# A fused kernel in twelve units of 256 rows in place of eight of 384

## What is computed

```python
k_n = k / (np.linalg.norm(k, axis=-1, keepdims=True) + 1e-06)
for t in range(S):                                  # 768 steps, for 4 x 8 heads
    y[:, :, t] = q[:, :, t] @ state
    v_old = state^T k_n[t]
    state = state + beta[t] * outer(k_n[t], v[t] - v_old)
x = y as rows of (4 * 768, 384)
x = (sigmoid(x @ w_gate) * (x @ w_val)) @ w_out     # 384 -> 1536 -> 384
out = x.copy()
rows with x @ w_skip > 0: e = argmax(x @ w_gate2)
    out = x + softmax(x @ w_gate2)[e] * (relu(x @ w1[e]) @ w2[e])   # 384 -> 1024 -> 384
```

## Time and profile before

| | |
|---|---|
| median of 3 runs | 981.93 us |
| profiled execution, its own time | 981.73 us |
| its span in the trace | 979.7 us |
| TensorE busy | 946.7 us (97%) |
| VectorE busy | 450.5 us (46%) |
| ScalarE busy | 165.1 us (17%) |
| GpSimd busy | 104.6 us (11%) |
| substitution on VectorE (L636, L638) | 79.2 + 79.8 us |
| dense products on TensorE (L1079, L1088, L1099) | 204.9 + 204.7 + 206.1 us |
| DMA over the span | 78.75 MB, mean 80 GB/s |

### The profile page before, as it was taken

The page is one execution under the profiler, slowest core; times in us unless marked ns, Lnnn a source line. Parts: engine busy times, 40 slices in busy tenths (PEclk is TensorE's granted clock), DMA queues, the critical chain, the costliest instruction groups (busy, mean ns, idle before and its releaser), DMA issues.

```text
span 979.7 us, 23053 instructions
## 1 busy us (share of the span) xinstructions
PE 946.7 (97%) x10087; PEld 629.2 (64%) x10087; DVE 450.5 (46%) x1100; ACT 165.1 (17%) x346; POOL 104.6 (11%) x136
## 2 busy tenths in 40 slices
PE   5999999999999999999999999999999999999995
PEld 5965655666565566566556655665555578878874
DVE  7967754766567457536753673212012211211121
ACT  2121211121121131122112111211110021111110
POOL 2010100011010010101010101001001222222221
PEclk9999999999999999999999999999999999999998
DMA  8830004003100400040031000000910115551400
GB/s 351 319 115 2 26 19 146 26 3 116 57 18 2 176 13 1 20 168 2 2 118 71 1 2 34 18 1 18 374 46 0 60 35 195 204 198 50 156 26 28
DMA packets 30299, 78.75 MB, mean 80 GB/s; under 512 B 4072, under 2 KB 20120, under 8 KB 29312
## 3 DMA queue, kind: packets, MB, share of 16 engines
q1 hardware_dynamic: 20112, 61.46, 17.2%
q10 hardware_dynamic: 6912, 9.55, 2.7%
q0 software_dynamic: 3184, 6.39, 2.2%
HBM read 65.34 MB, written 13.00 MB: 80 GB/s over the span
## 4 chain that ended last, share of the span: by engine, by line
PE 93%; DVE 2%; DMA 2%; issue 1%; POOL 1%; SPq 0%; ACT 0%; ACTq 0%; DVEq 0%; POOLq 0%
PE ps L1099 21%; PE ps L1079 19%; PE ps L1088 19%; PE ps L1152 9%; PE ps L1164 9%; PE ps L940 3%; PE ps L982 2%; PE ps L1038 2%; DMA prod<-in_turned_moe_w_out 1%; PE ps L1012 1%; PE ps L954 1%; PE ps L997 1%; PE ps L966 1%; PE ps L1027 1%; PE ps L1044 1%; PE ps L1137 1%
## 5 line engine op out<-in xcount | busy, mean ns | idle before, releaser
L1099 PE MATMUL ps<-wo,prod 128*128 128x393 f32 x576 | 206.1, 503 | 4.8 <-DVE prod L692 4.7
L1079 PE MATMUL ps<-xT,shared 128*128 128x384 f32 x576 | 204.9, 492 | 0.7 <-ACT xT L859 0.7
L1088 PE MATMUL ps<-xT,shared 128*128 128x384 f32 x576 | 204.7, 492 | 0.0
L692 DVE TENSOR_TENSOR prod<-sig,ps 128x384 f32<-128x384 f32 x96 | 52.9, 554 | 233.5 <-PE ps L1088 232.8
L1099 PEld LDWEIGHTS ps<-wo,prod 128*128 128x128 f32 x576 | 104.5, 189 | 76.5 <-DVE prod L692 8.6
L1079 PEld LDWEIGHTS ps<-xT,shared 128*128 128x128 f32 x576 | 106.7, 190 | 70.2 <-issue 0.8
L1088 PEld LDWEIGHTS ps<-xT,shared 128*128 128x128 f32 x576 | 106.9, 190 | 69.8
L1152 PEld LDWEIGHTS ps<-xgT,arena 128*128 128x128 f32 x816 | 93.7, 192 | 5.1 <-ACT xgT L887 0.8
L1152 PE MATMUL ps<-xgT,arena 128*128 128x128 f32 x816 | 94.0, 275 | 0.6 <-ACT xgT L887 0.6
L864 ACT ACTIVATE sig<-ps 128x384 f32<-128x384 f32 x96 | 47.1, 490 | 272.9 <-PE ps L1079 272.9
L1164 PE MATMUL ps<-arena,hT 128*128 128x384 f32 x272 | 90.5, 486 | 0.0
(11 more groups left out here) (171 smaller groups left out, 707.9 us busy)
## 6 DMA issues: line engine op xcount, KB each, us to landing
arena<-in_moe_w SPq DMA_DIRECT2D x16, 1536.0 KB, 10.6
arena<-in_kq SPq DMA_DIRECT2D x7, 1536.0 KB, 8.3
x_scratch<-x ACTq DMA_DIRECT2D x24, 196.5 KB, 4.1
arena<-in_kn SPq DMA_DIRECT2D x8, 576.0 KB, 4.8
shared<-in_v SPq DMA_DIRECT2D x8, 576.0 KB, 9.5
arena<-in_kr SPq DMA_DIRECT2D x8, 576.0 KB, 4.5
out<-x ACTq DMA_DIRECT2D x24, 192.0 KB, 4.2
prod<-in_turned_moe_w_out SPq DMA_DIRECT2D x1, 2304.0 KB, 12.9
```

Source lines behind the costliest of these rows:

```text
L692: nc.vector.tensor_tensor(prod[:, f, :], sig[:, f % 2, :], ps_m[3 - f % 2][:, 0:CT], ALU.mult)\
L1079: last = nc.tensor.matmul(ps_m[f % 2][:, 0:CT], wg[:, a, f * P:(f + 1) * P], xT[:, a, :], start=(a == 0), stop=(a == KT - 1))
L1088: last = nc.tensor.matmul(ps_m[3 - f % 2][:, 0:CT], wv[:, a, f * P:(f + 1) * P], xT[:, a, :], start=(a == 0), stop=(a == KT - 1))
L1099: last = nc.tensor.matmul(ps_m[t][:, 0:XW], prod[:, a, t * P:(t + 1) * P], wo[:, a, :], start=(a == 0), stop=(a == NF - 1))
```

## The change

A unit is now one chunk (JS = 1) of all four sequences (SEQ = 4), 256 rows; there are Q = 12 units, and one state runs through all of them. NS, the number of blocks in the lanes, goes from 24 to 16 of 32, and TT from 3 to 2. Each unit has one scan step with copies twice as wide. The Gram products of a unit stand in one burst (gk, then gq), x_turn is one burst. Keys for the norms have a tile of their own (`kn`) and no longer go through the lanes; the masking factors have one too (`fac`), and the diagonal blocks are copied into the lanes by four ScalarE copies in place of a ScalarE copy and a VectorE operation. The next substitution may begin right behind from_lanes, since the pieces of the order now carry costs in us, and what is left of a substitution when 18 us of dense pieces remain is given out at once. SyncE loads keys and queries on 48 partitions for each half, without padding.

The rows below are for one engine each, in its own order; "x3" is three equal instructions.

The diff, cut to its core:

```diff
-JS = 3
-SEQ = 2
+JS = 1
+SEQ = 4
-ROOT_MIN = 1e-15
+ROOT_MIN = 1e-30
+DENSITY = 0.8
+COST = {"gate": 1.29, "val": 1.29, "out": 2.03}
...
+    def follow(us):
+        owed[1] += us
+        while behind and owed[1] > 0:
+            event, w = behind.pop(0)
+            owed[1] -= w
+            order.append(event)
+        owed[1] = min(owed[1], 0.0)
+    def piece():
+        event = pieces.pop(0)
+        order.append(event)
+        us = COST.get(event[0], 0.0)
+        follow(DENSITY * us)
+        return us
+    def dense(us):
+        owed[0] += us
+        while pieces[0][0] != "x_turn" and (owed[0] > 0.5 or pieces[0][0] not in COST):
+            owed[0] -= piece()
+    def substitution(q):
+        return [(("turn_in", q, 0), 2.1)] +             [(("solve", q, u), 0.41 + 0.0021 * u * (H2 - 1 - u)) for u in range(1, H2 - 1)] + [(("from_lanes", q, 0), 5.3)]
...
+    order += [("norm", 0, 0), ("gk", 0, 0), ("lengths", 0, 0), ("mask", 0, 0), ("gq", 0, 0), ("mask", 0, 1)]
+    order += [("turn_in", 0, 0), ("router", 0, 0), ("gk", 1, 0), ("gq", 1, 0), ("warm", 0, 10)]
+    order += [event for event, _ in substitution(0)[1:]]
...
     for c in range(Q):
         q = c + 1
+        pieces += dense_pieces(c, Q, NF, TT)
         owed[0] = 0.0
         if q < Q:
+            if q + 1 < Q:
+                behind.insert(0, (("norm", q + 1, 0), 1.9))
+                dense(6.5)
+                order += [("gk", q + 1, 0), ("gq", q + 1, 0), ("pt", q + 1, 0)]
+                behind[0:0] = [(("lengths", q + 1, 0), 0.9), (("mask", q + 1, 0), 0.7), (("mask", q + 1, 1), 0.7)]
+            while ("from_lanes", q, 0) not in order:
+                if left() > 18.0:
+                    piece()
+                else:
+                    order.append(behind.pop(0)[0])
+            if q + 1 < Q:
+                behind += substitution(q + 1)
+            dense(2.2)
             order.append(("off", q, 0))
+            dense(1.9)
             order.append(("off", q, 1))
+            dense(1.9)
+            for stage in ("read", "apply", "write"):
+                order.append((stage, q, 0))
+                dense(1.6)
+        while pieces:
+            piece()
...
         load_kn(0)
-        load_first(0)
-        load_first(1)
-        load_first(2)
+        load_first(0, k_first)
         sp.dma_start(bt[:], beta_d).then_inc(beta_in, 16)
+        load_first(1, q_first)
...
         for q in range(2, Q):
             sp.wait_ge(y_done, JS * (q - 1))
+            load_kq(q)
+            load_kn(q)
             load_kr(q)
-            load_kq(q)
             load_v(q)
-            sp.wait_ge(dt_ready, q)
-            load_kn(q)
...
             elif stage == "turn_in":
+                if q:
+                    dve.wait_ge(dt_ready, q)
                 nc.vector.transpose(bl[:], bp[:])
...
+            elif stage == "gk":
+                act.wait_ge(gk_done, q + 1)
+                nc.scalar.activation(by_group(graw[:, q % 2]), grams(ps_a[:, 0:2]), ACT.Copy).then_inc(graw_copied, 1)
+                act.wait_ge(graw_copied, q + 1)
+                if q:
+                    act.wait_ge(turned_in, q)
+                for part in range(4):
+                    block = slice(H2 * part, H2 * (part + 1))
+                    last = nc.scalar.activation(dg[block, 0:NS, :], graw[block, q % 2, :, H2 * (part % 2):H2 * (part % 2 + 1)], ACT.Copy)
+                last.then_inc(dg_ready, 1)
...
+            if stage in ("gk", "gq"):
+                a = int(stage == "gq")
+                if q == 0:
+                    pe.wait_ge((k_first, q_first)[a], 32)
+                else:
+                    pe.wait_ge(kq_in[q % 2], 32 * ((q + 1) // 2))
...
             elif stage == "val":
                 if f >= 2:
                     pe.wait_ge(prod_ready, NF * q + f - 1)
-                elif f == 1 and q:
-                    pe.wait_ge(x2_copied, TT * q)
+                elif f == 0 and q >= 2:
+                    pe.wait_ge(rank_read, q - 1)
```

More of the change, by code:

```diff
@@ L50, in dense_pieces, with program_order @@
                 pieces += [(stage, q, 0) for stage in early.get((t, part), ())]
-            if t == TT - 1 and part < 3 and q + 1 < Q:
-                pieces.append(("x_turn", q + 1, part))
-    return pieces
-def program_order(Q, QS, NF, TT, KT):
-    light = ("route", "rank", "x_turn", "logits", "logit_turn")
-    order, pieces, later = [], [], []
+            if t == TT - 1 and part == 1 and q + 1 < Q:
+                pieces.append(("x_turn", q + 1, 0))
+    return pieces
+def program_order(Q, NF, TT):
+    order, pieces, behind = [], [], []
     owed = [0.0, 0.0]
[L66 to L69, removed]
+    def follow(us):
+        owed[1] += us
+        while behind and owed[1] > 0:
+            event, w = behind.pop(0)
             owed[1] -= w
@@ new lines, in program_order @@
+    order += [("turn_in", 0, 0), ("router", 0, 0), ("gk", 1, 0), ("gq", 1, 0), ("warm", 0, 10)]
+    order += [event for event, _ in substitution(0)[1:]]
+    order += [("router_copy", 0, 0), ("off", 0, 0), ("warm", 1, 1), ("pt", 0, 0), ("off", 0, 1), ("norm", 1, 0), ("warm", 1, 2)]
+    order += [("apply", 0, 0), ("warm", 1, 1), ("write", 0, 0), ("warm", 1, 1), ("x_turn", 0, 0), ("warm", 1, 2)]
+    order += [("lengths", 1, 0), ("mask", 1, 0), ("mask", 1, 1), ("pt", 1, 0)]
+    behind += substitution(1)
@@ L119, in program_order @@
             order.append(("off", q, 0))
-            dense(1.2)
+            dense(1.9)
             order.append(("off", q, 1))
[L122 to L126, removed]
-                dense(0.7)
-                later = prepare(q + 1)
-            steps = scan(q)
-            gap = max(0.7, (sum(p[0] not in light for p in pieces) - 4.0) / len(steps))
@@ L131, in program_order @@
-            for step in steps:
-                order.append(step)
-                dense(gap)
-        order += pieces
+            dense(1.9)
[4 more added lines that the diff above has]
+            piece()
     return order
@@ L309, in program @@
     kq_in = [sem(f"kq_in{i}") for i in range(2)]
-    kq_first = [sem(f"kq_first{i}") for i in range(3)]
+    k_first = sem("k_first"); q_first = sem("q_first")
     v_in = [sem(f"v_in{i}") for i in range(2)]
@@ new lines, in att @@
+                    pe.wait_ge((k_first, q_first)[a], 32)
+                else:
+                    pe.wait_ge(kq_in[q % 2], 32 * ((q + 1) // 2))
+                if q == 1:
+                    pe.wait_ge((graw_copied, raw_copied)[a], 1)
+                elif q and a == 0:
+                    pe.wait_ge(st_ready, writes(q - 2))
+                elif q:
+                    pe.wait_ge(xt_copied, q - 1)
+                for j in range(JU):
+                    for g in range(G2):
+                        for h in range(HH):
+                            n, to = ((G2 * j + g, h), (HH * j + h, g))[a]
+                            for c in range(CG):
+                                part = slice(GP * c, GP * c + D)
+                                last = nc.tensor.matmul(
+                                    ps_a[rows(to), 2 * a + c, n * C:(n + 1) * C], kq[part, q % 2, 0, j, g, h, :],
+                                    kq[part, q % 2, a, j, g, h, :], start=True, stop=True)
```

270 lines of the change are left out of this document (106 added, 164 removed).

## The result

The changed kernel takes 1000.48 us, the median of four runs from 999.11 to 1004.18, against 980.6 us for the kernel before (four runs of the same comparison, 978.76 to 982.52): a ratio of 1.021 with a 95% interval of 1.017 to 1.025. I had forecast 982.4 us, with 971 to 993 as the range: the time lies above the range, and "slower" had a chance of 0.26.

What follows compares the result with a forecast made beforehand. The order of TensorE's own work was taken to set the dense stretch. Start -15.7 and dense stretch +16.4 (work -4.9, waits and pace +21.3), end nothing, gave +0.7 on 981.73: 982.4 us, range 971 to 993.

Steps and rivals of the forecast that it cites:

- Unit 0's stop, 10.7: In unit 0, the output product waits for column block 11 behind substitution steps and leaving the lanes: 10.7 us.
- The off stops, 1.8, 1.4 and 1.9: In units 1 to 3, TensorE waits before the first off product while the lanes are left: together 5.1 us.
- Eleven seams, 11.5: Between value 11 and the first output, every seam waits for the last product: 0.74 or 1.25 each, 11.5 us.
- All waits together: In the dense stretch, unit 0, off and seam stops sum to 27.3 us against 8.0 before: +19.3.
- Slow pace after the stop, +2.0: After unit 0's stop, about 4 us of dense work run at half speed: +2.0 us (none to 4).
- Bursts, 0.4 us each, -12.4: In the dense stretch, bursts of small products fall from 106 to 75, at 0.4 us each: -12.4 us.
- small products: In the dense stretch, small-product records go from 5,978 to 6,406 at 14.5 ns each: +6.2 us.
- The start, -15.7: Before the first gate: fewer bytes, Gram and warm-up records and scan steps bring it to 52.2 us: -15.7.
- Rival 3: At the start, weights arrive as late and warm-up is all slow: -11.5 in place of -15.7, 986.6 us; chance 0.1.
- The end: nothing: From the last rank on, a list late by 1.5 us is hidden by the gather's wait for saved rows: nothing.
- Rival 1, the waits don't come: In the dense stretch, unit 0's stop, its restart and off stops are missing: 964.6 us, half 973.5; chance 0.22.
- Rival 2, VectorE bounds every unit: In mid-unit, VectorE falls behind and costs TensorE 1.3 us in each of ten units: 995.4 us; chance 0.18.

Runs made afterwards that it cites:

- experiment 2: Changed kernel with unit 0's threshold for the rest of the substitution loosened from 18.0 to 8.2 us: 1000.58 us, ratio 1.021.
- experiment 5: Changed kernel with the thresholds of both first units loosened, 8.2 us in unit 0 and 13.0 in unit 1: 994.9 us, ratio 1.013.
- experiment 6: Changed kernel with the output stage's first three quarters waiting for eleven products only, the last for the twelfth: 986.6 us, ratio 1.006.
- Experiment 4: Changed kernel with more dense work (3.9 for 2.2 us) ahead of the first off product in units 1 to 3: 995.24 us, ratio 1.016.
- experiment 7: Changed kernel with the Gram burst split in two, a dense piece between, in ten units: 1003.97 us, ratio 1.023.
- experiment 1: Changed kernel with all transposes of a turn ahead of all its products of halves, same instructions: 993.2 us, ratio 1.013.
- Experiment 3: Changed kernel with keys and queries padded to 128 partitions, one transfer in place of two on 48: 1000.29 us, ratio 1.020.
- experiment 8: Changed kernel with the edits of experiments 1, 4, 5 and 6 together: 973.11 us, ratio 0.992.
- experiment 9: Kernel of experiment 8 with the padded 128-partition loads of experiment 3 as well: 971.1 us, ratio 0.991.
- experiment 10: Kernel of experiment 9 with a dense piece ahead of each remaining wait and thresholds 9.5 and 14.5 us: 964.7 us, ratio 0.986.

## Why the prediction was wrong, point by point

- *Unit 0's stop, 10.7.* Right: 10.06 idle, at the place and put down to the operation that was named. Experiments 2, 5 and 6 show that the block of steps ahead of the last product makes it.
- *The off stops, 1.8, 1.4 and 1.9.* Right: 4.9 in three (said: 5.1). Experiment 4 takes 3.8 of it away.
- *Eleven seams, 11.5.* Too high: 8.8. The steady one waits 0.97, which is 1.14 with its loss of pace (604.58 to 607.01, less a piece of 1.295), where I had 1.25. My sum had a slip too: five at 0.74 and six at 1.25 are 11.2. The mechanism (three steps ahead of the last product) is seen in experiment 7, whose steady unit has two there and waits 0.61.
- All waits together: said +19.3 (27.3 with their pace, against 8.0), measured +18.6 of idle time. **So the waits aren't what was missed.**
- *Slow pace after the stop, +2.0.* Right for the first: 4.16 us (100.12 to 104.28) for the 2.09 behind a steady seam (607.01 to 609.10), +2.1. Not foreseen: the short stops can have it too. Behind the stop of 1.65 in unit 1 the two off bursts and the value piece between them took 1.6 us more (5.20 from 154.57 to 159.77, for 3.62 from 575.70 to 579.32).
- *Bursts, 0.4 us each, -12.4.* A little high: 0.36 by experiment 7, so -11.2 for 31: +1.2, of which 0.8 without the turn bursts.
- *The turn burst.* **This is the step that failed**, inside the terms "small products" and "bursts". I took its records at the 14.5 ns of all small products and its burst price at the 0.4 us of the others; by that, ten bursts fewer save 4.0 us and twelve records more cost 0.2, so -3.8. Measured: 21 bursts took 13.1 us before and eleven take 20.5 now, +7.4. The forecast is short by 11.2 us here. With the kinds of record sorted the eleven take 11.0 (experiment 1), so 9.5 of the 11.2 come from the alternation inside the burst, which the full diff and the kernel show and to which no row of before that I had taken gives a price. Before, the bursts held one form each, and moving them together brought the forms side by side. Why the sorted burst still takes 1.7 us more in all than my prices give isn't settled.
- *The start, -15.7.* It came out at -11.4, and "I am wrong if the first gate comes after 56" has happened, at 56.47. The router started 5.2 us later than said (20.19 for 15.0). I had counted fewer bytes at the old rate of 424 GB/s; the rate was 230 from 12 to 20 us. Experiment 3 gives back 3.7 of the 5.2 with more bytes on more partitions. The warm-up was 2.1 shorter than said (4.5 us for 6.6), and from off to the first gate it took 12.6 and not 11.5, of which 0.9 is the turn burst. Rival 3 had -11.5 as its price, with the chance 0.1. That it is so near to -11.4 is luck: it had the weights as late as before and a warm-up that is all slow, and they came 2.9 us later than before, with a warm-up at full pace from its second record on.
- *The end: nothing.* Right: 8.9 us from the last output record to the first expert product, before (776.12 to 785.03) and after (795.03 to 803.90).
- *Rival 1, the waits don't come:* refuted. *Rival 2, VectorE bounds every unit:* no value piece waited for a product; the only other waits for VectorE in the dense stretch are two before apply products, of 1.0 us together. Its 995.4 lies nearer to the result than the forecast does, for another reason.

The sum again, as errors of the forecast: turn +11.2, start +4.3, second slow stretch +1.6, burst price of the other bursts +0.8, waits -0.7. That is 17.2 of the 17.9 us between 982.4 and the profiled 1000.29; the rest isn't settled.

Two slips in the chances change little: added up from the rivals, faster comes to 0.23 and slower to 0.28, where I wrote 0.25 and 0.26, and rival 2 stands at 995.4, above the 993 that was to take in most of it.

On the clock, the trace spoke for the pace. In the dense layer the granted-clock row shows the drop: 0.51 of 2.4 GHz, near the lower level of 1.2 GHz, behind the stop of unit 0. At the start its 1.00 is no reading of the clock: the trace's list of clock levels begins only at 42.38 us before and at 39.34 us after, and the view prints 1.00 where the list has nothing. The pace changes at just these marks. Before, the warm-up records start 0.43 us apart until 42.17 and 0.22 apart from 42.49 on. After, the Gram burst up to 39.33 takes 29 ns a record, and the warm-up behind it 0.22 us a record.

## What to carry to other kernels

When bursts of small matmuls are put together, look at what stands beside what: the same records in sorted order took half the time. Price a transfer by the rate of its own shape, not by its bytes at the rate of its neighbours. And before a stop is hidden by moving work, ask what the waiting instruction reads: a wait for eleven of twelve products gave back more than any edit of the order, and it was worth 4 us in the old kernel too.

## What the runs showed of the hardware that I had not expected

- A transpose of 64 rows onto 128 and a product onto 64 that follow each other start 0.15 to 0.20 us apart, two of one form 0.06 to 0.11 (from one pair to the next). Whether it is the change of form or the write to the other columns of the same bank wasn't tested apart.
- The DMA engines, busy all the time, moved 230 GB/s with two transfers of 48 partitions in the mix, and 415 with one of 128 in their place.
- Stops of 1.4 to 1.9 us were followed by some 3 to 7 us at a granted clock of 0.5 in six of the eleven traces of the changed kernel and its variants (units 1 to 5), and not always: experiments 8 to 10 have such stops, of up to 1.7 us, and no slow stretch behind them. In experiments 2 and 5 a slow stretch also stands in unit 0 behind two stops of 0.93 and 1.08 us, and experiments 8 to 10 have the same two stops without it. What decides it is open. The stop of 10 us had it in all five traces that have it, and the stops of 6.0 and 6.9 us (experiments 6 and 2) had it too.
